# Step 2's W_in split placed behind step 1's activations, and the last two units' value products placed behind step 0's seventh product

## The chip, the cores and the metric

The kernel runs on one core of a Trainium2 chip. The metric is the device time of one execution in microseconds (us), the median of several runs. Its engines are called PE (TensorE, matmuls), ACT (ScalarE), DVE (VectorE), POOL (GpSimd) and SP (SyncE, which here only issues transfers).

## The reference

Three parts follow each other, all in fp32.

1. Banded attention: 2 batches x 8 heads, 768 positions, head size 64. A query sees the first 8 positions and the last 96 up to itself, with a distance bias; softmax; product with V.
2. `x1 = silu(x @ W_in) @ W_out` on 1536 tokens, model width 512, hidden width 2048.
3. `x2 = (h * clip(h + 3, 0, 6) / 6) @ W_out2` with `h = x1 @ W_in2`, same sizes. The output is 1536 x 512.

## The kernel before, in words

Every engine has its own hand-written list of instructions, executed in that order; semaphores order the lists against each other. An instruction that waits holds up all that stands behind it on its engine.

**Attention.** Eight pairs of heads x 6 query tiles give 48 *units* (`NU = 48`). For a unit PE computes scores (`scores`, line 901), DVE subtracts and finds the maximum, ACT exponentiates, POOL multiplies by the inverse sum, PE transposes (`turn_probs`, 911), DVE or ACT copies the transposed tile out of PSUM (`copy_t`), and PE multiplies with V (`values`, 926). `values(u)` waits for the copy of unit `u`. Every third unit ACT copies the result into `x_raw` (`x_copy`, 702; the last one, `x_copy(15)`, waits for `values` of units 45 to 47).

**The two feed-forward layers.** There are 32 *steps* (`NSTEP`): four blocks (layer, batch) of 8 steps, each step handling 256 of 2048 hidden columns for 768 tokens. In a step the product with W_in is done by a seven-product (Winograd form of Strassen's) scheme: POOL makes four sums of quarters of the weights (`w_sum`, lines 300, 302, 305, 308), and PE runs the products in the order P1, P2, P6, P5, P7, P3, P4 (`product`, line 954). Every fp32 operand is cut into a high part (ACT, a copy to fp32r) and a low part (DVE, a subtraction), and each product is 6 matmuls of 128x384: hi x hi, lo x hi, hi x lo, for two halves of the depth. So a step has 42 of them. Two PSUM banks hold the partial results (`p_bank`):

- `keep` (ACT, line 728) copies P1 out to `p1_c`, P6 to `u2_c`, P5 to `p5_c`. P6 waits for `p1_c`; P7, which adds into the bank that `u2_c` is read from, waits for `u2_c`; P3 waits for `p5_c`.
- `c_sum` (DVE, 478) adds such a copy to a bank: first after P2, then after P7, then after P3. P5 waits for the first, P4 for the second.
- `gated` (ACT, 740) takes the sigmoid of four quarters, `silu` (DVE, 488) multiplies; `g_high` (ACT, 821) and `g_low` (DVE, 607) cut the result in two; `down` (PE, 1022 and 1023) multiplies with W_out in 48 matmuls per step, one step later: after the products of step `s` PE runs `down(s-1, 0)` and `down(s-1, 1)`.
- `w_high(s, part)` (ACT, 709, 128x896) and `w_low(s, part)` (DVE, 463) cut the weights of step `s` and their sums, in two parts. `w_high(s, .)` waits for all four `w_sum`s of its step. P1 of step `s` waits for the second `w_low(s, 1)` and for the four `silu`s of the step before. The load of the weights of step `s + 2` (SP) waits for `w_low(s, 1)` too.
- `wo_high` (ACT, 748) and `wo_low` (POOL, 336, 128x1024) cut W_out. POOL's list after attention is `wo_low(0)`, which waits for the fourth `silu` of step 0, `w_sum` of step 2 (four), `w_sum` of step 3 (four), `wo_low(1)`, `w_sum` of step 4, `wo_low(2)`, and so on.

**The places that the change touches.** Steps 0 and 1 have their weights cut during attention. Step 2 is the first one whose weights are cut in the general loop, and its first part stands by itself: behind `keep(1, p1_c)` on ACT (`w_high(2, 0)`), and behind `g_low(0, 1)` on DVE (`w_low(2, 0)`). The second parts stand behind the activations of step 1. In the function `banded` of PE the end of attention is woven into step 0:

```
turn_probs(NU - 1)
values(NU - 2)
for n in range(P6, P4 + 1):
    product(0, n)
values(NU - 1)
```

Of the kernel before, what the change touches and what calls it, by code (L numbers as in the profile page):

```python
# [16 lines left out]
NU = NPAIR * NT  # L17
# [41 lines left out]
def at_least(eng, sem, value):  # L59

    if isinstance(value, int) and value <= 0:
        return
    eng.wait_ge(sem, value)


def build(nc, qT, kT, v, w_in1, w_out1, w_in2, w_out2, counts, out):
    outer = ExitStack()
    with outer:
# [72 lines left out]
        def o_bank(g): return ps[:, g % 2, 0:TB]  # L141
# [254 lines left out]
        def _(dve):  # L396
# [62 lines left out]
            def w_low(s, part):  # L459

                at = slice(7 * P * part, 7 * P * part + 7 * P)
                dve.wait_ge(wi_hi_ok, 2 * s + part + 1)
                nc.vector.tensor_tensor(wi_lo[:, s % 2, at], wi_raw[:, s % 2, QC + 7 * P * part:QC + 7 * P * part + 7 * P],  # L463
                                        wi_hi[:, s % 2, at], ALU.subtract).then_inc(wi_lo_ok, 1)
# [9 lines left out]
            def c_sum(s, i, bank, add, product):  # L474

                dve.wait_ge(p_done, 7 * s + product + 1)
                dve.wait_ge(kept, 3 * s + {0: 1, 1: 3, 2: 3}[i])
                nc.vector.tensor_tensor(c_sb[:, i, :], p_bank(bank), add[:, :], ALU.add).then_inc(c_ok, 1)  # L478
# [5 lines left out]
            def silu(s, n):  # L484

                dve.wait_ge(gate_ok, 4 * s + n + 1)
                at_least(dve, g_hi_ok, 2 * s)
                nc.vector.tensor_tensor(g_quad(n), h_quad(n), gate[:, n, :], ALU.mult).then_inc(g_ok, 1)  # L488
# [113 lines left out]
            def g_low(s, f):  # L602

                dve.wait_ge(g_hi_ok, 2 * s + f + 1)
                src, hi, lo = g_f[:, f, :, :].rearrange("p a t -> p (a t)"), g_hi[:, s % 2, f, :], g_lo[:, s % 2, f, :]
                if s < NSTEP // 2:
                    nc.vector.tensor_tensor(lo, src, hi, ALU.subtract).then_inc(g_lo_ok, 1)
                else:
                    nc.vector.scalar_tensor_tensor(lo, src, 1.0 / 6.0, hi, ALU.mult, ALU.subtract).then_inc(g_lo_ok, 1)
# [22 lines left out]
            for s in range(1, NSTEP):  # L632
                blk, f = s // STEPS, s % STEPS
                evict = blk > 0 and f == 1
                c_sum(s, 0, 1, p1_c, P2)
                if s == 1:
                    g_low(0, 1)
                    w_low(2, 0)
                if evict:
                    w_low(s + 1, 1)  # L640
                    y_copy(blk - 1, 5)
                c_sum(s, 1, 0, p5_c, P7)
                c_sum(s, 2, 1, u2_c, P3)
                for n in range(4):
                    if s < NSTEP // 2:
                        silu(s, n)
                    else:
                        hswish(s, n)
                g_low(s, 0)
                g_low(s, 1)  # L650
                if s == 1:
                    w_low(2, 1)
                if f == STEPS - 1 and s < NSTEP - 1:
                    for i in range(7):
                        x_low(blk + 1, i)
                if s + 2 < NSTEP:
                    w_low(s + 2, 0)
                    if blk > 0 and f == 0:
                        y_copy(blk - 1, 1)
                        y_copy(blk - 1, 3)  # L660
                    else:
                        w_low(s + 2, 1)
# [7 lines left out]
        def _(act):  # L670
# [33 lines left out]
            def w_high(s, part):  # L704

                at = slice(7 * P * part, 7 * P * part + 7 * P)
                act.wait_ge(ws_ok, 4 * s + 4)
                at_least(act, p_done, 7 * (s - 1))
                nc.scalar.activation(wi_hi[:, s % 2, at], wi_raw[:, s % 2, QC + 7 * P * part:QC + 7 * P * part + 7 * P],  # L709
                                     ACT.Copy).then_inc(wi_hi_ok, 1)  # L710
# [130 lines left out]
            for s in range(1, NSTEP):  # L841
                blk, f = s // STEPS, s % STEPS
                evict = blk > 0 and f == 1
                keep(s, p1_c, 0, P1)
                if s == 1:
                    w_high(2, 0)
                if evict:
                    w_high(s + 1, 1)
                    y_copy(blk - 1, 2)
                if s > 1:  # L850
                    wo_high(s)
                keep(s, u2_c, 0, P6)
                keep(s, p5_c, 1, P5)
                if evict:
                    y_copy(blk - 1, 4)
                for n in range(4):
                    gated(s, n)
                g_high(s, 0)
                g_high(s, 1)
                if s == 1:  # L860
                    w_high(2, 1)
                if f == STEPS - 1 and s < NSTEP - 1:
                    for i in range(7):
                        x_high(blk + 1, i)
                if s + 2 < NSTEP:
                    w_high(s + 2, 0)
                    if blk > 0 and f == 0:
                        y_copy(blk - 1, 0)
                    else:
                        w_high(s + 2, 1)  # L870
# [7 lines left out]
        def _(pe):  # L878
# [36 lines left out]
            def values(u):  # L915
                it, t = u // NT, u % NT
                if u % 3 == 0:
                    at_least(pe, x_ok, u // 3 - 1)
                if t == 0:
                    pe.wait_ge(v_in[it % 2], 16 * (it // 2 + 1))  # L920
                pe.wait_ge(*copied(u))
                o = o_bank(u // 3)
                for a in range(0 if t else 1, 2):
                    for h in range(2):
                        vv = v_raw[it % 2][:, h, t if a else NT + t - 1, :]
                        mm = nc.tensor.matmul(o[D * h:D * h + D, P * (t % 3):P * (t % 3) + P], vv,  # L926
                                              probsT[:, u % 2, 2 * h + a, :], start=(a == 0 or t == 0), stop=(a == 1))
                mm.then_inc(pv_done, 1)

            def product(s, n):  # L930

                a, b, bank = PRODUCTS[n]
                if n == P1:
                    pe.wait_ge(wi_lo_ok, 2 * s + 2)
                    at_least(pe, g_ok, 4 * s)
                elif n == P2:
                    at_least(pe, c_ok, 3 * s)
                elif n == P6:
                    pe.wait_ge(kept, 3 * s + 1)
                elif n == P5:  # L940
                    pe.wait_ge(c_ok, 3 * s + 1)
                elif n == P7:
                    pe.wait_ge(kept, 3 * s + 2)
                elif n == P3:
                    pe.wait_ge(kept, 3 * s + 3)
                elif n == P4:
                    pe.wait_ge(c_ok, 3 * s + 2)
                if s % STEPS == 0:
                    pe.wait_ge(x_lo_ok, 7 * (s // STEPS) + b + 1)
                fresh = n in (P1, P2, P5)  # L950
                for k in range(2):
                    at = slice(QC * a + P * k, QC * a + P * k + P)
                    for i, (w, x) in enumerate(((wi_hi, x_hi), (wi_lo, x_hi), (wi_hi, x_lo))):
                        mm = nc.tensor.matmul(p_bank(bank), w[:, s % 2, at], x[:, b, k, :],  # L954
                                              start=fresh and k == 0 and i == 0, stop=k == 1 and i == 2,
                                              skip_group_check=True)
                mm.then_inc(p_done, 1)

            def banded():
                for u in range(NU):  # L960
                    scores(u)
                    if u >= LAG:
                        turn_probs(u - LAG)
                    if u >= LAG + 1:
                        values(u - LAG - 1)
                values(NU - 6)
                turn_probs(NU - 5)
                pe.wait_ge(neg_done, 2 * NU)
                product(0, P1)
                turn_probs(NU - 4)  # L970
                values(NU - 5)
                product(0, P2)
                turn_probs(NU - 3)
                values(NU - 4)
                turn_probs(NU - 2)
                values(NU - 3)
                turn_probs(NU - 1)
                values(NU - 2)
                for n in range(P6, P4 + 1):
                    product(0, n)  # L980
                values(NU - 1)

            def general():
# [84 lines left out]
            s = NSTEP - 1  # L1068
# [53 lines left out]
```

## Time and profile before

| | |
|---|---|
| median of 3 runs | 608.09 us (607.88 to 610.44) |
| the profiled execution, its own time | 607.72 us |
| its span, first to last instruction | 606.0 us |
| mean granted PE clock | 0.997 |
| PE busy | 594.7 us (98%) |
| DVE busy | 369.2 us (61%) |
| ACT busy | 341.6 us (56%) |
| POOL busy | 284.1 us (47%) |

Times in the trace count from the start of the span. Attention reaches to about 95 us, step 0 lies between 88 and 101 us, step 1 from 102.7 us; from there on the steps follow each other, and PE is busy in nearly all of each slice.

### The profile page before, as it was taken

What the parts mean: (1) busy time and instruction counts of PE and PEld (TensorE: products, weight loads), DVE (VectorE), ACT (ScalarE), POOL (GpSimd) and SP (SyncE); (2) the same over time, 40 slices, a digit from 0 to 9 for tenths busy, and PEclk for the clock granted to TensorE, in tenths of its full rate; (3) what the DMA queues carried; (4) which work ended last, traced back from release to release, by engine and by line L of the source; (5) the groups of instructions that cost most, each with busy time, mean ns of one, the idle gap of its engine ahead of it and who ended that gap; (6) DMA issues with size and microseconds to landing.
All of it is one profiled execution on the core that took longest, in us unless ns stands there. A gap on an engine that the chain in (4) does not pass through costs nothing.

```text
span 606.0 us, 9614 instructions
## 1 busy us (share of the span) xinstructions
PE 594.7 (98%) x3429; PEld 516.4 (85%) x3429; DVE 369.2 (61%) x696; ACT 341.6 (56%) x659; POOL 284.1 (47%) x353
## 2 busy tenths in 40 slices
PE   8999999799999999999999999999999999999998
PEld 5665568799999999999999998888888988898896
DVE  6678886655755568557555865575557685554331
ACT  6889885544454466444444675545447565555441
POOL 4787995656933314439433144394333343331110
PEclk9999999899999999999999999999999999999999
DMA  8435330032222113221211123212221252221002
GB/s 351 162 110 206 110 117 5 34 138 70 71 70 70 70 35 105 70 69 37 88 59 64 38 70 101 71 36 104 70 69 36 70 175 70 69 70 35 1 1 104
DMA packets 14595, 50.05 MB, mean 83 GB/s; under 512 B 1618, under 2 KB 1874, under 8 KB 14546
## 3 DMA queue, kind: packets, MB, share of 16 engines
q1 hardware_dynamic: 14258, 48.63, 23.4%
q10 hardware_dynamic: 288, 0.79, 0.4%
q8 instruction: 28, 0.46, 0.3%
q14 instruction: 21, 0.17, 0.1%
HBM read 46.27 MB, written 3.15 MB: 82 GB/s over the span
## 4 chain that ended last, share of the span: by engine, by line
PE 88%; POOL 6%; ACT 2%; DVE 2%; issue 1%; DMA 0%; DVEq 0%; ACTq 0%
PE ps L954 38%; PE ps L1031 22%; PE ps L1022 14%; PE ps L1023 8%; POOL probs L291 3%; PE ps L926 2%; PE ps L911 2%; PE ps L901 2%; POOL rsume L283 1%; ACT probs L680 1%; POOL wo_lo L336 0%; POOL x_t L323 0%; POOL x_t L328 0%; DVE x_lo L472 0%; DVE g_f L488 0%
## 5 line engine op out<-in xcount | busy, mean ns | idle before, releaser
L336 POOL TENSOR_TENSOR wo_lo<-wo_raw,wo_hi 128x1024 fp32r<-128x1024 f32 x32 | 76.6, 2395 | 265.7 <-ACT wo_hi L748 258.3
L954 PE MATMUL ps<-x_hi,wi_hi 128*128 128x384 f32 x448 | 151.6, 338 | 4.1 <-ACT u_c L728 3.1
L954 PE MATMUL ps<-x_hi,wi_lo 128*128 128x384 f32 x448 | 150.6, 336 | 0.0
L954 PE MATMUL ps<-x_lo,wi_hi 128*128 128x384 f32 x448 | 150.4, 336 | 0.0
L478 DVE TENSOR_TENSOR c_sb<-ps,p_c 128x384 f32<-128x384 f32 x64 | 35.6, 557 | 166.4 <-PE ps L954 166.1
L728 ACT ACTIVATE p_c<-ps 128x384 f32<-128x384 f32 x64 | 31.5, 492 | 132.3 <-PE ps L954 132.1
L954 PEld LDWEIGHTS ps<-x_hi,wi_hi 128*128 128x128 f32 x448 | 84.6, 189 | 8.0 <-ACT u_c L728 4.3
L954 PEld LDWEIGHTS ps<-x_hi,wi_lo 128*128 128x128 f32 x448 | 84.5, 189 | 0.7
L954 PEld LDWEIGHTS ps<-x_lo,wi_hi 128*128 128x128 f32 x448 | 84.5, 189 | 0.0
L1031 PE MATMUL ps<-wo_hi,g_lo 128*128 128x512 f32 (+1 forms) x194 | 76.3, 393 | 0.0
L1031 PE MATMUL ps<-wo_lo,g_hi 128*128 128x512 f32 (+1 forms) x194 | 76.3, 393 | 0.0
L1031 PE MATMUL ps<-wo_hi,g_hi 128*128 128x512 f32 (+1 forms) x194 | 76.2, 393 | 0.0
L463 DVE TENSOR_TENSOR wi_lo<-wi_raw,wi_hi 128x896 fp32r<-128x896 f32 x64 | 72.4, 1166 | 3.1 <-ACT wi_hi L709 3.1
L821 ACT ACTIVATE g_hi<-g_f 128x768 fp32r<-128x768 f32 x64 | 50.6, 838 | 37.1 <-DVE g_f L488 21.3
L709 ACT ACTIVATE wi_hi<-wi_raw 128x896 fp32r<-128x896 f32 x64 | 57.4, 938 | 4.9 <-POOL wi_raw L308 4.9
L1022 PE MATMUL ps<-g_hi,wo_hi 128*128 128x512 f32 x128 | 50.0, 391 | 0.0
L1022 PE MATMUL ps<-g_lo,wo_hi 128*128 128x512 f32 x128 | 50.0, 391 | 0.0
L1022 PE MATMUL ps<-g_hi,wo_lo 128*128 128x512 f32 x128 | 50.0, 390 | 0.0
L680 ACT ACTIVATE probs<-negs,negmax 128x256 f32<-128x256 f32 (+1 forms) x96 | 45.9, 481 | 5.5 <-DVE negmax L499 5.2
L291 POOL TENSOR_SCALAR probs<-probs,rinv 128x256 f32<-128x256 f32 (+1 forms) x96 | 45.3, 485 | 4.1
L499 DVE CUSTOM_DVE_ANT_0 negs<-ps,m_bias 128x256 f32<-128x256 f32 (+1 forms) x96 | 37.3, 391 | 14.7 <-PE ps L901 12.1
L1031 PEld LDWEIGHTS ps<-wo_hi,g_lo 128*128 128x128 f32 x194 | 36.4, 188 | 8.6
(94 smaller groups left out, 1091.0 us busy)
## 6 DMA issues: line engine op xcount, KB each, us to landing
wi_raw<-in_w_in SPq DMA_DIRECT2D x32, 512.0 KB, 3.3
wo_raw<-in_w_out SPq DMA_DIRECT2D x32, 512.0 KB, 3.4
v_raw<-in_v SPq DMA_DIRECT2D x8, 704.0 KB, 4.2
k_raw<-in_kT SPq DMA_DIRECT2D x8, 464.0 KB, 5.0
out_y<-y_out SPq DMA_DIRECT2D x11, 256.0 KB, 4.4
q_raw<-in_qT SPq DMA_DIRECT2D x6, 384.0 KB, 5.5
q_raw<-in_qT ACTq DMA_DIRECT2D x2, 384.0 KB, 4.0
out_y<-y_out SPq DMA_DIRECT2D x2, 128.0 KB, 1.9
```

The costliest lines, as they stand in the source:

```text
L291: nc.gpsimd.tensor_scalar(probs[:, u % DEEP, h, a:256], probs[:, u % DEEP, h, a:256], rinv[:, u % DEEP, h:h + 1], 1.0, ALU.mult, ALU.mult) ...
L336: nc.gpsimd.tensor_tensor(wo_lo[:, s % 2, :], wo_raw[:, s % 2, :], wo_hi[:, s % 2, :], ALU.subtract).then_inc(wo_lo_ok, 1)
L463: nc.vector.tensor_tensor(wi_lo[:, s % 2, at], wi_raw[:, s % 2, QC + 7 * P * part:QC + 7 * P * part + 7 * P], wi_hi[:, s % 2, at], ALU.sub ...
L478: nc.vector.tensor_tensor(c_sb[:, i, :], p_bank(bank), add[:, :], ALU.add).then_inc(c_ok, 1)
L499: nc.vector.tensor_tensor_reduce(negs[:, u % 2, h, 0 if t else P:256], sc, bi, -0.125, 3.0e38, ALU.add, ALU.min, negmax[:, u % DEEP, h:h + ...
L680: nc.scalar.activation(probs[:, u % DEEP, h, a:256], negs[:, u % 2, h, a:256], ACT.Exp, bias=negmax[:, u % DEEP, h:h + 1], scale=-1.0, acc ...
L709: nc.scalar.activation(wi_hi[:, s % 2, at], wi_raw[:, s % 2, QC + 7 * P * part:QC + 7 * P * part + 7 * P], ACT.Copy).then_inc(wi_hi_ok, 1)
L821: nc.scalar.activation(g_hi[:, s % 2, f, :], g_f[:, f, :, :].rearrange("p a t -> p (a t)"), ACT.Copy, scale=1.0 if s < NSTEP // 2 else 1.0 ...
L954: mm = nc.tensor.matmul(p_bank(bank), w[:, s % 2, at], x[:, b, k, :], start=fresh and k == 0 and i == 0, stop=k == 1 and i == 2, skip_grou ...
L1022: nc.tensor.matmul(y_bank(i), wo[:, s % 2, w], g[:, s % 2, c, 0:512], start=first, stop=last)
L1023: mm = nc.tensor.matmul(y_bank(4 + i // 2)[:, 256 * (i % 2):256 * (i % 2) + 256], wo[:, s % 2, w], g[:, s % 2, c, 512:S], start=first and ...
L1031: mm = nc.tensor.matmul(y_bank(t)[:, cols], g[:, s % 2, c, P * t:P * t + P], wo[:, s % 2, DM * c + cols.start:DM * c + cols.stop], start=s ...
```

## The change

On ACT `w_high(2, 0)`, and on DVE `w_low(2, 0)`, move from the middle of step 1 to behind the `g_high`s and `g_low`s of step 1, directly ahead of `w_high(2, 1)` and `w_low(2, 1)`. On PE `values(46)` moves from ahead of P6 of step 0 to behind P4 of step 0, ahead of `values(47)`. Nothing is added or removed.

```
@@ DVE
                 c_sum(s, 0, 1, p1_c, P2)
                 if s == 1:
                     g_low(0, 1)
-                    w_low(2, 0)
...
                 g_low(s, 0)
                 g_low(s, 1)
                 if s == 1:
+                    w_low(2, 0)
                     w_low(2, 1)
@@ ACT
                 keep(s, p1_c, 0, P1)
-                if s == 1:
-                    w_high(2, 0)
...
                 g_high(s, 0)
                 g_high(s, 1)
                 if s == 1:
+                    w_high(2, 0)
                     w_high(2, 1)
@@ PE, banded
                 turn_probs(NU - 1)
-                values(NU - 2)
                 for n in range(P6, P4 + 1):
                     product(0, n)
+
+                values(NU - 2)
                 values(NU - 1)
```

ACT in steps 0 and 1 (`g_high` of step 0 first; p_c is `p1_c` or `p5_c`, u_c is `u2_c`):

```order
 L821 ACTIVATE g_hi<-g_f 128x768 x2
 L728 ACTIVATE p_c<-ps 128x384
-L709 ACTIVATE wi_hi<-wi_raw 128x896
-L728 ACTIVATE u_c<-ps 128x384
-L728 ACTIVATE p_c<-ps 128x384
-L740 ACTIVATE gate<-c_sb 128x384 x3
-L740 ACTIVATE gate<-ps 128x384
-L821 ACTIVATE g_hi<-g_f 128x768 x2
-L709 ACTIVATE wi_hi<-wi_raw 128x896 x3
+L728 ACTIVATE u_c<-ps 128x384
+L728 ACTIVATE p_c<-ps 128x384
+L740 ACTIVATE gate<-c_sb 128x384 x3
+L740 ACTIVATE gate<-ps 128x384
+L821 ACTIVATE g_hi<-g_f 128x768 x2
+L709 ACTIVATE wi_hi<-wi_raw 128x896 x4
```

The copies `u2_c` and `p5_c` of step 1 now come directly behind `p1_c`, and four weight cuts (two for step 2, two for step 3) follow step 1's `g_high`s instead of three.

DVE in step 1, from its first `c_sum` on:

```order
 L478 TENSOR_TENSOR c_sb<-ps,p_c 128x384
 L607 TENSOR_TENSOR g_lo<-g_f,g_hi 128x768
-L463 TENSOR_TENSOR wi_lo<-wi_raw,wi_hi 128x896
-L478 TENSOR_TENSOR c_sb<-ps,p_c 128x384
-L478 TENSOR_TENSOR c_sb<-ps,u_c 128x384
-L488 TENSOR_TENSOR g_f<-c_sb,gate 128x384 x3
-L488 TENSOR_TENSOR g_f<-ps,gate 128x384
-L607 TENSOR_TENSOR g_lo<-g_f,g_hi 128x768 x2
-L463 TENSOR_TENSOR wi_lo<-wi_raw,wi_hi 128x896 x3
+L478 TENSOR_TENSOR c_sb<-ps,p_c 128x384
+L478 TENSOR_TENSOR c_sb<-ps,u_c 128x384
+L488 TENSOR_TENSOR g_f<-c_sb,gate 128x384 x3
+L488 TENSOR_TENSOR g_f<-ps,gate 128x384
+L607 TENSOR_TENSOR g_lo<-g_f,g_hi 128x768 x2
+L463 TENSOR_TENSOR wi_lo<-wi_raw,wi_hi 128x896 x4
```

The subtraction for step 2's first part leaves the place ahead of step 1's second `c_sum` and stands first of four behind the `g_low`s.

## Rows read from the trace of the kernel before

**Rows 1.** Waits of PE, whole span: line, releaser, us in total, times, longest us
```profile
PE ps L954 <- ACT u_c L728: 3.1, 1, 3.1
PE ps L911 <- POOL probs L291: 2.3, 7, 0.7
...
PE ps L954 <- DVE g_f L488: 0.7, 1, 0.7
...
PE ps L954 <- DVE c_sb L478: 0.3, 1, 0.3
```

**Rows 2.** Timeline of PE: start us, us, line, operation, [idle before, releaser]
```profile
103.80 0.33 PE L954 MATMUL ps<-x_hi,wi_hi 128*128 128x384 f32 x1
...
106.35 0.44 PE L954 MATMUL ps<-x_hi,wi_hi 128*128 128x384 f32 x1 [0.31 <-DVE c_sb L478]
...
110.72 0.69 PE L954 MATMUL ps<-x_hi,wi_hi 128*128 128x384 f32 x1 [3.05 <-ACT u_c L728]
...
115.32 0.39 PE L1022 MATMUL ps<-g_hi,wo_hi 128*128 128x512 f32 x1
...
123.66 0.34 PE L954 MATMUL ps<-x_hi,wi_hi 128*128 128x384 f32 x1
```

**Rows 3.** Timeline of ACT, steps 0 and 1
```profile
102.00 0.49 ACT L702 ACTIVATE x_raw<-ps 128x384 f32<-128x384 f32 x1
103.99 0.49 ACT L728 ACTIVATE p_c<-ps 128x384 f32<-128x384 f32 x1
109.34 0.95 ACT L709 ACTIVATE wi_hi<-wi_raw 128x896 fp32r<-128x896 f32 x1 [4.85 <-POOL wi_raw L308]
110.20 0.47 ACT L728 ACTIVATE u_c<-ps 128x384 f32<-128x384 f32 x1
```

**Rows 4.** Timeline of POOL, steps 0 to 1
```profile
102.61 2.40 POOL L336 TENSOR_TENSOR wo_lo<-wo_raw,wo_hi 128x1024 fp32r<-128x1024 f32 x1 [7.35 <-DVE g_f L488]
104.97 1.44 POOL L300 TENSOR_TENSOR wi_raw<-wi_raw 128x256 f32<-128x256 f32 x1
108.58 0.72 POOL L308 TENSOR_TENSOR wi_raw<-wi_raw 128x256 f32<-128x256 f32 x1
```

**Rows 5.** Busy time of each engine by stretch (100 to 120 us)
```profile
105.00:110.00 5.00, 2.36 (x12) 1.72 (x11) 2.23 (x3) 0.66 (x1) 4.92 (x7) 1.00 0.30 105
110.00:115.00 5.00, 4.28 (x17) 4.28 (x18) 2.37 (x4) 1.99 (x5) 4.92 (x4) 0.66 0.00 0
```

**Rows 6.** Timeline of PE, end of step 0
```profile
101.02 0.34 PE L954 MATMUL ps<-x_lo,wi_hi 128*128 128x384 f32 x1
101.29 0.66 PE L926 MATMUL ps<-probsT,v_raw 128*64 128x128 f32 x8
102.68 0.41 PE L954 MATMUL ps<-x_hi,wi_hi 128*128 128x384 f32 x1 [0.73 <-DVE g_f L488]
```

**Rows 7.** Timeline of DVE, end of step 0 and step 1
```profile
101.98 0.55 DVE L488 TENSOR_TENSOR g_f<-ps,gate 128x384 f32<-128x384 f32 x1
103.32 2.50 DVE L607 TENSOR_TENSOR g_lo<-g_f,g_hi 128x768 fp32r<-128x768 f32 x1 [0.79 <-ACT g_hi L821]
105.75 0.55 DVE L478 TENSOR_TENSOR c_sb<-ps,p_c 128x384 f32<-128x384 f32 x1
```

**Rows 8.** Timeline of DVE, from the last matmuls of step 1
```profile
114.96 1.76 DVE L488 TENSOR_TENSOR g_f<-c_sb,gate 128x384 f32<-128x384 f32 x3
119.37 3.09 DVE L463 TENSOR_TENSOR wi_lo<-wi_raw,wi_hi 128x896 fp32r<-128x896 f32 x3
130.57 2.33 DVE L488 TENSOR_TENSOR g_f<-c_sb,gate 128x384 f32<-128x384 f32 x3
```

**Rows 9.** By source line: duration ns min/median/max, first and last start us
```profile
L607 DVE TENSOR_TENSOR g_lo<-g_f,g_hi x32: 946/959/2504, 103.3 to 338.1; 128x768 fp32r<-128x768 f32 x32
L488 DVE TENSOR_TENSOR g_f<-c_sb,gate x48: 544/736/1375, 99.8 to 335.7; 128x384 f32<-128x384 f32 x48
L463 DVE TENSOR_TENSOR wi_lo<-wi_raw,wi_hi x64: 1075/1085/1904, 38.7 to 559.6; 128x896 fp32r<-128x896 f32 x64
```

More of the change, by code:

```diff
@@ L637, in _ @@
                     g_low(0, 1)
-                    w_low(2, 0)
                 if evict:
@@ L651, in _ @@
                 if s == 1:
+                    w_low(2, 0)
                     w_low(2, 1)
@@ L844, in _ @@
                 keep(s, p1_c, 0, P1)
-                if s == 1:
-                    w_high(2, 0)
                 if evict:
@@ L860, in _ @@
                 if s == 1:
+                    w_high(2, 0)
                     w_high(2, 1)
@@ L977, in banded @@
                 turn_probs(NU - 1)
-                values(NU - 2)
                 for n in range(P6, P4 + 1):
                     product(0, n)
+                values(NU - 2)
                 values(NU - 1)
```

## Prediction

> **What bounds the kernel now.** I read the totals first: PE is busy 98% of the span, the next engine 61%. So the end is set by PE's list, and a change can only matter through PE's idle time, its clock, or new waits. The list of PE's waits comes next [rows 1]. It is short. The largest single wait of the whole run is one of 3.1 us: a matmul of the W_in products that waits for ACT's copy `u2_c`. One of 0.7 us waits for a `silu`. The 2.3 us at line 911 are seven small waits inside attention, which the change doesn't touch.
>
> The timeline of PE puts the long wait into step 1 [rows 2]. P2 of step 1 starts at 103.80, P5 at 106.35, and the next product, P7, only at 110.72. ACT shows why [rows 3]: `u2_c` needed only P6, whose six matmuls ended at about 106.0, but its copy ran at 110.20, because `w_high(2, 0)` stood ahead of it in ACT's list, ran at 109.34, and had itself been waiting 4.85 us for POOL. POOL had begun only at 102.61, with `wo_low(0)`, and finished the fourth sum of step 2 at 108.58 + 0.72 = 109.30 [rows 4]. So the chain is POOL, `w_high(2, 0)`, `u2_c`, P7, and nobody needs `w_high(2, 0)` before P1 of step 2, at 123.66 [rows 2].
>
> The view by stretches adds a second cost [rows 5]: in 105 to 110 us PE works 2.36 of 5 us at granted clock 1.00; in 110 to 115 us the clock is 0.66 on average, full (2.4 GHz) for part and half (1.2 GHz) for part. The stretch that follows the idle time is run partly at the low level.
>
> **Edit A, `w_high(2, 0)` and `w_low(2, 0)` moved.** Three terms.
>
> 1. The idle time. P5 to P7 takes 110.72 - 106.35 = 4.37 us. Six matmuls at the usual distance take 1.04 us (P2 started 1.04 us before P6), 1.15 us with the slower first one behind a wait. Gain: 4.37 - 1.15 = 3.2 us. Is anything else late at P7? `u2_c` now follows P6 directly, as ACT has nothing between: about 106.1 to 106.6, ahead of P7's new turn. P3 wants `p5_c`, a copy of 0.49 us behind P5, with a whole product for it. P4 wants the second `c_sum`, one product after P7; DVE is free by then, since `w_low(2, 0)` has left that place as well.
> 2. The clock. From P7 to the first `down` matmul there are 18 matmuls: 115.32 - 110.72 = 4.60 us [rows 2]. At 1.04 us for six they take 3.12 us. Gain: 1.5 us, since with no long idle time there is nothing that the clock would fall after.
> 3. What the moved work costs in its new place. Two instructions: 0.95 us on ACT [rows 3], 1.08 us on DVE [rows 9]. PE's next use is P1 of step 2, which waits for `w_low(2, 1)`. Between P4 of step 1 and P1 of step 2 PE has `down` of step 0: 123.66 - 115.32 = 8.34 us [rows 2]. Before, DVE came to `w_low(2, 1)` at 119.37 and ended it about 1.03 us later (3.09 us for three) [rows 8], that is 120.4, or 5.1 us behind the start of `down`. With one more subtraction it is 6.1 us: 2.2 us before PE asks. That is the bound with no loss.
>
> But term 3 has a second bound. DVE's subtractions and products that read two SBUF tiles stretch where POOL is at work: `g_low` takes 0.96 us in the median and took 2.50 us at 103.32, ending at 105.82, 0.8 us behind the end of `wo_low(0)` at 105.0 [rows 4, 7]; the `silu`s go up to 1.38 us from 0.54, and `w_low` to 1.90 from 1.08 [rows 9]. Additions that read PSUM keep 0.55 us. With step 1 now ending five microseconds earlier, its `silu`s and `g_low`s fall on POOL's sums for step 3 and on `wo_low(1)`, which before ran mostly while DVE was idle. I lay POOL's list out from its new start (edit B): `wo_low(0)` at 102.0, sums of step 2 to 108.7, sums of step 3 to about 112.1 (two of them held up by DVE), `wo_low(1)` (2.40 us) to about 114.9. DVE: `silu`s from 109.7 in about 2.8 us (2.33 us for three in step 2, under the same kind of load [rows 8]), the fourth to 113.0, ACT's `g_high`s to 114.2. The first `g_low` then waits for `wo_low(1)` to end, as it did for `wo_low(0)`: 115.7; the second 116.5; two `w_low`s to 118.5 to 118.8. PE would be ready for P1 at 110.0 + 8.34 = 118.4. I take a wait of **0.3 us**, since the layout leaves it between 0 and 0.6. If every one of the seven SBUF-only operations (three `silu`, two `g_low`, two `w_low`) were stretched as far as the longest rows [rows 9], it would be 3 x 0.83 + 2 x 1.54 + 2 x 0.82 = 7.2 us, a wait of 5 us, and the low clock once more behind it. That is the far bound, and it is not near: POOL has only one 2.4 us operation there.
>
> The Trainium skill ("SBUF — State Buffer", section "Who interferes with whom") says that a DVE instruction with two SBUF inputs and a GpSimd instruction that reads SBUF take one shared port in turn, each for its whole length. The trace agrees: `g_low` at 103.32 ended 0.8 us after `wo_low(0)` did. It is this rule that speaks against the change; without it the wait at P1 would be nil and the sum 0.3 us better.
>
> **What else hangs on the moved operations.** The load of step 4's weights follows `w_low(2, 1)`; before, that ended 3.2 us ahead of step 2's P1, now at about the same time as P1. So POOL gets to the sums of step 4 and to `wo_low(2)` some 3 us later within step 2, where the `silu`s of step 2 meet them. The first user is P1 of step 4, two steps later, and `down(2)`, over a step later; I cost it at nothing. The cover is POOL's idle time, about half the span (47% busy).
>
> **Edit B, `values(46)` behind P4.** It takes 0.59 us of PE's time wherever it stands: the last P4 matmul starts at 101.02, `values(47)` at 101.29 and ends at 101.95, and P1 of step 1 at 102.68 after 0.73 us of waiting for the fourth `silu` of step 0, which ran 101.98 to 102.53 [rows 6, 7]. With `values(46)` behind the products, all five products and the `silu`s that follow them come 0.59 us earlier; the `silu` ends at 101.94, `values(47)` at 101.95 as before. P1 starts at 102.1. The wait was swapped for work: 0.6 us. Does it last? Not all of the way on ACT: `x_copy(15)` still waits for `values(47)`, so it stays at 102.00, and `p1_c` of step 1 behind it at 103.99 [rows 3]. P6 waits for that to 104.6 (P2 ends at 104.2). The next gate is P5, which waits for the `c_sum` at 105.75 on DVE [rows 7]. It stood behind the long `g_low`, and this one behind `wo_low(0)` on POOL, which is released by the very `silu` that comes 0.59 us earlier. So P5 starts at 105.8 for 106.35: **0.6 us**, with 0.1 us to spare at P6. Bounds: 0 (P6 or ACT takes it) and 0.7.
>
> **Sum.** 3.2 + 1.5 + 0.6 - 0.3 = 5.0 us. The profiled execution took 607.72 us with a span of 606.0; it becomes 602.7 with a span of 601.0. The median of the runs shown is 0.37 us above the profiled one, so I forecast 608.09 - 5.0 = **603.1 us**. After P1 of step 2 everything moves along: the list of waits holds none of PE that the next steps would bring back [rows 1].
>
> **Rivals.**
>
> 1. *The port takes more.* POOL's `wo_low(1)` catches a `silu` as well as a `g_low`, or the `w_low`s too, and P1 of step 2 waits 1 to 2.5 us. For: the stretched rows [rows 9]; against: one such operation in the window. Gain 5.3 - 1.8 = 3.5, 604.6 us (603.8 to 605.3).
> 2. *Edit B is swallowed.* `x_copy(15)` and the copies behind it hold up P6 so that P5 is not earlier. Gain 4.4, 603.7 us. The range holds it.
> 3. *The low clock was not in the timed runs.* The clock fell in the profiled execution after 3.2 us of idling. If it did not in the median run, that run can only gain the idle time: 3.2 + 0.6 - 0.3 = 3.5 us, 604.6. For: nothing in the rows; against: its time agrees with the median within 0.1%. The Trainium skill ("TensorE: Matmul & The Clock Gate", section "What's actually happening") says that the point of transition depends on where in the monitor's window the matmuls fall and varies from run to run; no single trace can show it.
> 4. *Slower.* P1 of step 2 waits so long that PE loses the clock there. Place: `w_low(2, 1)`, behind ACT's four cuts and the stretched DVE operations. Price: the wait plus 1.5 us. It decides from 3.8 us of waiting on, as 3.8 + 1.5 = 5.3: `w_low(2, 1)` ending later than 122.2. The far bound of 5 us gives 608.09 - 5.3 + 6.5 = 609.3. For it: only the far bound; against it: in my layout it ends at 118.5 to 118.8.
> 5. *The change doesn't do what it says.* Something else releases P7 late, so that the idle time stays. Against: `u2_c` ran directly behind `w_high(2, 0)`, with P6 4 us done. Then only edit B is left: 607.5 us.
>
> **How the numbers follow.** Forecast (with rival 2 in its range) 0.75, rival 1 0.12, rival 3 0.06, rival 4 0.03, rival 5 0.04. A measurement of this kernel can tell about 0.5%, 3.0 us, from no change. Faster by more than that is below 605.05: the forecast, rival 3 and most of rival 1, 0.91. Within 0.5%: the rest of rival 1, rival 5, some of rival 4, 0.07. Slower by more than 0.5% (over 611.1): 0.02. The range runs from 602.0 (no wait at P1, 0.7 from edit B, and 0.7 us of spread between runs) to 605.3, where rival 1 ends.
>
> **What would show it.** In the profile of the changed kernel: no wait of PE for `u2_c` at step 1, and granted clock 1.00 from 105 to 115 us; P5 of step 1 at 105.8, the first `down` matmul at 110.0, for 106.35 and 115.32; a new short wait of PE for `wi_lo` (DVE, line 463) at about 118.4, with `g_low` of step 1 stretched beside `wo_low(1)`; and no new one later. Wrong: a wait over 1 us there (rival 1), a clock below 1 around 120 us (rival 4), or P7 still behind P5 by more than 1.2 us (rival 5).

## The result and the profile after

The changed kernel took 604.42 us (median of 11 runs, 602.71 to 606.27), the kernel before in the same set 608.14 us (11 runs, 606.59 to 610.57); the ratio is 0.9927, with a 95% interval of 0.9908 to 0.9946. That is 3.7 us between the medians, 4.4 us by the ratio. The profiled execution took 604.96 us, with a span of 603.2 us and a mean granted clock of 0.994. The forecast was 603.1 us, with a range of 602.0 to 605.3.

The waits of PE in the changed kernel, whole span (line, releaser, us in total, times, longest):

```profile
PE ps L910 <- POOL probs L291: 2.8, 6, 1.4
PE ps L884 <- POOL ident L276: 1.4, 1, 1.4
PE ps L900 <- DVE negmax L499: 1.2, 3, 0.7
PE ps L900 <- DMA k_raw<-in_kT: 0.4, 1, 0.4
PE ps L953 <- DVE g_f L488: 0.3, 1, 0.3
```

The wait of 3.1 us for `u2_c` [rows 1] is gone, and the 0.7 us for the `silu` is 0.3. The 1.2 us at line 900 (scores) is new; it lies in early attention, where the change does nothing, and is taken up below.

PE's timeline (line 953 is 954 of before), in the places of [rows 2, 6]:

```profile
102.91 1.10 PE L925 MATMUL ps<-probsT,v_raw 128*64 128x128 f32 x16
104.29 0.41 PE L953 MATMUL ps<-x_hi,wi_hi 128*128 128x384 f32 x1 [0.29 <-DVE g_f L488]
...
107.98 0.44 PE L953 MATMUL ps<-x_hi,wi_hi 128*128 128x384 f32 x1
...
109.13 0.33 PE L953 MATMUL ps<-x_hi,wi_hi 128*128 128x384 f32 x1
...
112.25 0.39 PE L1022 MATMUL ps<-g_hi,wo_hi 128*128 128x512 f32 x1
...
120.84 0.44 PE L953 MATMUL ps<-x_hi,wi_hi 128*128 128x384 f32 x1
```

These are both `values`, then P1, P5 and P7 of step 1, `down` of step 0, and P1 of step 2. P7 follows P5 after 1.15 us (4.37 before), `down` follows P7 after 3.12 us (4.60 before). P1 of step 2 stands 8.59 us behind the start of `down`, for 8.34 before: the new wait, 0.25 us. The granted clock is 1.00 in every stretch from 100 to 125 us.

ACT, DVE and POOL in step 1 [rows 3, 4, 7, 8]:

```profile
105.99 0.47 ACT L728 ACTIVATE p_c<-ps 128x384 f32<-128x384 f32 x1
107.88 0.49 ACT L728 ACTIVATE u_c<-ps 128x384 f32<-128x384 f32 x1 [1.42 <-PE ps L953]
...
116.34 3.46 ACT L709 ACTIVATE wi_hi<-wi_raw 128x896 fp32r<-128x896 f32 x4
```

```profile
105.38 2.07 DVE L607 TENSOR_TENSOR g_lo<-g_f,g_hi 128x768 fp32r<-128x768 f32 x1 [1.24 <-ACT g_hi L821]
107.38 0.55 DVE L478 TENSOR_TENSOR c_sb<-ps,p_c 128x384 f32<-128x384 f32 x1
...
111.88 2.94 DVE L488 TENSOR_TENSOR g_f<-c_sb,gate 128x384 f32<-128x384 f32 x3
114.74 0.55 DVE L488 TENSOR_TENSOR g_f<-ps,gate 128x384 f32<-128x384 f32 x1
115.73 3.06 DVE L607 TENSOR_TENSOR g_lo<-g_f,g_hi 128x768 fp32r<-128x768 f32 x2 [0.44 <-ACT g_hi L821]
118.71 4.08 DVE L463 TENSOR_TENSOR wi_lo<-wi_raw,wi_hi 128x896 fp32r<-128x896 f32 x4
```

```profile
104.23 2.41 POOL L336 TENSOR_TENSOR wo_lo<-wo_raw,wo_hi 128x1024 fp32r<-128x1024 f32 x1 [6.57 <-DVE g_f L488]
...
114.37 2.73 POOL L336 TENSOR_TENSOR wo_lo<-wo_raw,wo_hi 128x1024 fp32r<-128x1024 f32 x1
```

`u2_c` waits for PE now, not for a place in ACT's list. On DVE the three `silu`s take 2.94 us and the two `g_low`s 3.06 us beside POOL's sums and `wo_low(1)`, which itself is stretched from 2.40 to 2.73 us. The second `w_low` ends at about 118.71 + 2.06 = 120.77, and P1 follows at 120.84.

So the places that the change touches look as forecast, yet the span is 603.2 us and not 601.0. Where the rest went shows in the first 20 us. The stretches 10 to 15 and 15 to 20 us, of before and of after (PE, PEld, DVE, ACT and POOL busy, granted clock, DMA):

```profile
10.00:15.00 5.00, 4.11 (x26) 2.03 (x24) 3.64 (x21) 5.00 (x22) 3.24 (x10) 1.00 1.03 410
15.00:20.00 5.00, 5.00 (x50) 3.13 (x46) 3.35 (x17) 4.30 (x15) 3.72 (x11) 1.00 0.47 180
```

```profile
10.00:15.00 5.00, 3.56 (x16) 1.85 (x16) 2.31 (x15) 4.76 (x21) 3.35 (x10) 0.68 1.02 411
15.00:20.00 5.00, 5.00 (x29) 2.93 (x28) 2.69 (x11) 2.45 (x8) 3.17 (x8) 0.63 0.44 168
```

In the profiled execution of the changed kernel the clock was at its lower level for part of early attention, and PE got through 29 instructions in the second stretch where it did 50 before. P1 of step 0 starts at 91.09 us, against 88.69 before. That is 2.4 us which no instruction of the change explains: up to there both kernels run the same list.

The two executions differ from the first scores on. Before:

```profile
5.48 6.17 PE L901 MATMUL ps<-k_raw,q_raw 64*128 64x256 f32 x24 [0.31 <-DMA k_raw<-in_kT]
```

After:

```profile
5.57 1.14 PE L900 MATMUL ps<-k_raw,q_raw 64*128 64x256 f32 x8 [0.41 <-DMA k_raw<-in_kT]
...
12.14 0.69 PE L910 MATMUL ps<-ident,probs 128*128 128x128 f32 x2 [1.40 <-POOL probs L291]
12.77 1.22 PE L900 MATMUL ps<-k_raw,q_raw 64*128 64x256 f32 x4
```

In the changed kernel's execution the first scores ran faster, PE then had to wait for DVE's `negmax` (the 1.2 us at line 900) and for POOL, and the clock fell at about 12 us. In the execution of before the scores ran slowly without a gap, and no fall came.

This gives a cleaner measure: the time from P1 of step 0 to the end of the span. It was 606.0 - 88.69 = 517.3 us before and 603.2 - 91.09 = 512.1 us after, 5.2 us less. (Spans are given to 0.1 us, so this measure is good to about that.)

### The profile page after: what moved, and what is told of

The parts are those of the page before. It is cut to its first block, busy times and chain, and to the rows that moved or that the text cites. A ratio compares the mean times of both kernels' runs of the same rounds, so it can differ in the third digit from the quotient of the medians.

```text
span 603.2 us, 9614 instructions
## 1 busy us (share of the span) xinstructions
PE 593.7 (98%) x3429; PEld 515.2 (85%) x3429; DVE 373.6 (62%) x696; ACT 341.5 (57%) x659; POOL 284.3 (47%) x353
## 4 chain that ended last, share of the span: by engine, by line
PE 89%; DVE 4%; POOL 3%; ACT 2%; issue 1%; DMA 0%; DVEq 0%; ACTq 0%
PE ps L953 38%; PE ps L1031 22%; PE ps L1022 14%; PE ps L1023 7%; PE ps L910 3%; PE ps L900 3%; PE ps L925 3%; POOL probs L291 2%; ACT probs L680 1%; POOL rsume L283 1%; DVE g_lo L607 1%; DVE wi_lo L463 1%; DVE g_f L488 0%; DVE x_lo L472 0%; POOL x_t L328 0%
```

## The experiments

The theory was the prediction's sum: 3.2 us of idle time and 1.5 us of lower clock in step 1 (edit A), 0.6 us at the seam of attention (edit B), 0.3 us given back at P1 of step 2; and, from the profile after, that early attention varies from execution to execution for reasons of its own. The rivals were that the two edits need each other, that the slow matmuls of step 1 have another cause than the wait, that DVE's half of edit A matters, and that P1 of step 2 had slack left.

The profiled execution of each kernel gives the same measures (us; the start of the first matmul of the product named, from the PE timeline):

| kernel | P1 of step 0 | P1 of step 1 | P5 | P7 | P1 of step 2 | span | span less P1 of step 0 |
|---|---|---|---|---|---|---|---|
| before | 88.69 | 102.68 | 106.35 | 110.72 | 123.66 | 606.0 | 517.3 |
| changed | 91.09 | 104.29 | 107.98 | 109.13 | 120.84 | 603.2 | 512.1 |
| changed, again | 88.90 | 102.10 | 105.78 | 106.96 | 118.62 | 601.0 | 512.1 |
| edit A alone | 89.15 | 103.12 | 106.80 | 107.97 | 119.63 | 602.0 | 512.9 |
| edit B alone | 88.98 | 102.19 | 105.87 | 110.25 | 123.39 | 605.7 | 516.7 |
| `w_low` half of A | 91.82 | 105.77 | 109.44 | 113.81 | 126.93 | 609.2 | 517.4 |
| before, wait filled | 88.69 | 102.64 | 106.31 | 110.68 | 122.27 | 604.5 | 515.8 |
| before, early fill | 92.93 | 106.88 | 110.56 | 114.92 | 128.90 | 611.2 | 518.3 |
| changed, early fill | 89.07 | 102.26 | 105.94 | 107.12 | 118.78 | 601.2 | 512.1 |
| changed, `w_low` delayed | 88.75 | 101.94 | 105.61 | 106.76 | 120.48 | 604.8 | 516.1 |
| changed, POOL reordered | 91.17 | 104.37 | 107.57 | 108.61 | 121.07 | 603.5 | 512.3 |
| changed, POOL spaced | 90.11 | 103.30 | 106.50 | 107.53 | 118.99 | 601.9 | 511.8 |

P1 of step 0 moves between 88.7 and 92.9 us, and not with the edits: the changed kernel has 91.09 in one execution and 88.90 in another. The last column is steady: 512.1 twice for the changed kernel. Steadier still is the time from P1 of step 2 to the end, 482.3 us before (606.0 - 123.66) and 482.4 in both executions of the changed kernel, so that all of the 5.2 us lies between P1 of step 0 and P1 of step 2.

**Edit A alone.** The four hunks on DVE and ACT of the change, with the values left in place.

> Edit A alone: the two weight cuts of step 2 moved, the values left where they were. My theory (three terms: idle time 3.2 us, low clock 1.5 us, a short wait at P1 of step 2 of 0.2 us): P7 of step 1 follows P5 within 1.2 us, the first down matmul of step 0 comes 4.7 us earlier relative to P5, and the time is 4.4 us below the kernel before when early attention runs at the same clock in both. A rival, that the two edits only work together (the cuts moved without the earlier silu leave POOL's sums late for something else), would show another wait of PE in step 1 and less than 3 us of gain.

Measured: 603.71 us (6 runs, 603.31 to 606.09), before 609.13 (22 runs), ratio 0.9914 (0.9893 to 0.9936). By the last column 517.3 - 512.9 = 4.4 us, as expected. P7 follows P5 after 1.17 us. The edit works by itself; the rival falls. The medians are 5.4 us apart, more than for the whole change, because four of the six runs had the quick start (mean clock 1.000); the last column is free of that.

**Edit B alone.** The hunk on PE of the change.

> Edit B alone: values of unit 46 behind P4, the cuts left in place. My theory: P1 of step 1 starts 0.6 us earlier, and POOL's list too, so that w_high(2, 0), u2_c and P7 all come 0.6 us earlier (P7 is released by POOL's chain, which starts at the fourth silu): 0.6 us less in all, the low clock of step 1 stays. The rival, that x_copy(15) and p1_c hold it back: less than 0.2 us. In the timed comparison neither can be told from nothing; the trace tells.

Measured: 607.34 us (11 runs, 606.94 to 610.47), ratio 0.9975 (0.996 to 0.999). By the last column 0.6 us less. `x_copy(15)` did not hold it back. P1 of step 1 still waits 0.3 us for the `silu`, where the prediction had no wait left. P7 is still late:

```profile
102.19 0.41 PE L954 MATMUL ps<-x_hi,wi_hi 128*128 128x384 f32 x1 [0.29 <-DVE g_f L488]
105.87 0.44 PE L954 MATMUL ps<-x_hi,wi_hi 128*128 128x384 f32 x1 [0.15 <-DVE c_sb L478]
110.25 0.45 PE L954 MATMUL ps<-x_hi,wi_hi 128*128 128x384 f32 x1 [3.07 <-ACT u_c L728]
```

From P1 of step 0 to P5 it saves 17.66 - 16.89 = 0.77 us, a little more than the 0.6 forecast: besides the 0.59 us of `values(46)`, P6 starts 0.41 us behind the start of the last transposes, where `values(46)` started 0.58 us behind it. At P7 there is 22.03 - 21.27 = 0.76 us; behind P7 the lower clock comes at another place, and 0.6 is left at the end.

**The wait filled with other work.** On PE, between P5 and P7 of step 1 of the kernel before:

```
                     for n in range(7):
                         product(s, n)
+                        if s == 1 and n == P5:
+                            for _ in range(18):
+                                nc.tensor.transpose(ps[:, 2, 0:P], ident[:, :], ident[:, :])
```

> The kernel before, order untouched, with 18 unused 128x128 transposes on PE between P5 and P7 of step 1, into a bank that nothing reads at that time. They fill 2.7 us of the 3.1 us in which PE waits for u2_c, and change nothing of the wait itself. My theory (the wait costs 1.5 us more than its own length, because the clock falls after it): P7 still starts 4.4 us behind P5, but the 18 matmuls from P7 to the first down matmul take 3.1 to 3.2 us instead of 4.6, granted clock 1.00 in 105 to 120 us, and the fastest runs are 1.3 to 1.5 us below the fastest of the kernel before. The rival, that the slow matmuls have another cause (transfers, the pile-up of copies on ACT and DVE): 4.6 us as before and no gain.

Measured: 607.44 us (12 runs, 606.21 to 609.16), before 608.86 (23 runs, 606.43 to 612.11), ratio 0.9982 (0.9965 to 0.9998). The wait stands, 1.1 us of it unfilled, and the clock stays up:

```profile
110.68 0.45 PE L954 MATMUL ps<-x_hi,wi_hi 128*128 128x384 f32 x1 [1.10 <-ACT u_c L728]
```

```profile
105.00:110.00 5.00, 4.28 (x30) 3.69 (x28) 2.18 (x3) 0.70 (x1) 4.92 (x6) 1.00 0.30 105
110.00:115.00 5.00, 4.32 (x25) 4.19 (x26) 3.76 (x4) 2.89 (x7) 4.92 (x4) 1.00 0.01 3
```

The 18 transposes filled 2.0 us, less than the 2.7 expected. P7 starts 4.37 us behind P5, to the hundredth as before, so nothing of the wait itself was removed; from P7 to `down` it is 113.94 - 110.68 = 3.26 us for 4.60, and the last column falls by 1.5 us. This is the clock [rows 5], the second term of edit A, measured by itself: 1.3 us up to `down`, 1.5 us at the end. The fastest run, 606.21 us, is only 0.2 us below the fastest of before in this set (606.43) and 1.3 us below the next (607.55). The run also gives the span that the kernel before has when it keeps the clock in step 1: 604.5 to 604.7 us. Five of the 12 filled runs have that, and one of the 23 of before, 604.6 us at a mean clock of 0.999; in all sets together two of 67 runs of before took less than 607 us. Other runs of before may have kept the clock in step 1 and lost it in early attention: the filled kernel then has spans of 605.6 to 606.0 us, which can't be told from before with the loss in step 1 (605.8 to 606.3).

**DVE's half of edit A.** Only `w_low(2, 0)` moved on DVE, `w_high(2, 0)` left on ACT.

> Half of edit A: only DVE's w_low(2, 0) moved behind the g_lows of step 1, ACT's w_high(2, 0) left in the middle of step 1. My theory (ACT's list is what holds P7: u2_c stands behind w_high(2, 0)): P7 still 4.4 us behind P5, PE's 3.1 us wait for u2_c stays. From P7 on, DVE's second c_sum of step 1 comes 0 to 0.3 us sooner; no other difference. The rival, that DVE's subtraction was part of the hold-up: P7 or P4 a microsecond earlier.

Measured: one execution only, 610.95 us, span 609.2 with a late start of step 0 at 91.82; the last column is 517.4 for 517.3. PE still waits 3.05 us for `u2_c`:

```profile
113.81 0.44 PE L954 MATMUL ps<-x_hi,wi_hi 128*128 128x384 f32 x1 [3.05 <-ACT u_c L728]
```

P7 is 4.37 us behind P5. So DVE's half does nothing by itself, and what holds P7 is in ACT's list. ACT's half alone was not run: `w_low(2, 0)` waits for `w_high(2, 0)`, so DVE would then stand at its old place until the cut was made.

**P1 of step 2 delayed.** The changed kernel with, on DVE:

```
                 if s == 1:
                     w_low(2, 0)
+                    for j in range(2):
+                        nc.vector.tensor_tensor(y_out[:, 2 * j:2 * j + 2, 0:448],
+                                                wi_raw[:, 0, QC:QC + 7 * P].rearrange("p (a k) -> p a k", a=2),
+                                                wi_raw[:, 0, QC:QC + 7 * P].rearrange("p (a k) -> p a k", a=2), ALU.subtract)
                     w_low(2, 1)
```

> The changed kernel with two unused subtractions of 128x896 on DVE (1.02 us each, results into the output buffer, overwritten at the end) between w_low(2, 0) and w_low(2, 1). My theory (P1 of step 2 is now released by w_low(2, 1), with no slack left): P1 of step 2 starts 2.0 us later than in the changed kernel, PE waits 2.2 us for DVE line 463, and the time rises by 2.0 us, or by up to 3.5 if the clock falls behind the wait. The rival, that P1 had slack of about 2 us and the 0.2 us gap there was something else: no wait over 0.5 us and the time unchanged.

Measured: 605.84 us (10 runs, 604.89 to 607.81), ratio to before 0.995 (0.9928 to 0.9972). The profile shows the wait with its name, and the clock that went with it:

```profile
120.48 0.69 PE L957 MATMUL ps<-x_hi,wi_hi 128*128 128x384 f32 x1 [2.10 <-DVE wi_lo L463]
```

```profile
120.00:122.00 2.00, 1.52 (x5) 1.52 (x6) 2.00 (x3) 0.00 (x0) 0.00 (x0) 0.62 0.28 109
122.00:124.00 2.00, 2.00 (x8) 2.00 (x7) 0.43 (x1) 1.20 (x2) 0.43 (x1) 0.53 0.87 336
```

From P1 of step 0 to P1 of step 2 it is 31.73 us, for 29.72 to 29.75 in the changed kernel: the added 2.0 us in full. So `w_low(2, 1)` is what releases P1, without slack. Five of the ten runs kept the clock (mean 1.000) and have spans of 603.1 to 603.4 us, 2.1 to 2.4 over the 601.0 of the changed kernel at that clock. The profiled one lost it behind the wait, and paid 516.1 - 512.1 = 4.0 us in all, more than the 3.5 that I had set as the upper end: the lower clock took 2.0 us here. So a wait of 2 us costs the clock in some executions and not in others.

**Early attention filled.** For the kernel before, and the same for the changed one:

```
                 for u in range(NU):
                     scores(u)
+                    if 1 <= u < 5:
+                        busy(2)
+                    if u == 5:
+                        busy(6)
```

> The kernel before with added PE work in early attention: two unused 128x128 transposes behind the scores of units 1 to 4, six behind those of unit 5, all into a bank that nothing reads yet. They fill idle time of PE between 7 and 12 us. My theory on the spread between runs (602.7 to 606.3 for the changed kernel, by the mean granted clock 1.000 to 0.994): in some executions the clock falls to its lower level in early attention, where PE idles, which has nothing to do with the change. With the idle time filled it should stay high: runs no longer at 610 us, median 606.5 to 608. The rival, that the spread comes from elsewhere: the same spread and median as the kernel before, or up to 1 us more for the added work.

> The changed kernel with the same added PE work in early attention. My theory: nearly all runs at the level of the fastest of the changed kernel, 602.7 us, with clock 1.000; the difference to the kernel before with the same filling is then the whole of the forecast, 4.5 to 5.2 us (less if that one loses no clock in step 1 in its median run: then 3.7). The rival: 604.4 us with the old spread.

Measured: 609.38 us for before with the filling (12 runs, 607.5 to 613.17), ratio 1.0004 (0.9983 to 1.0026); 604.3 us for the changed kernel with it (6 runs, 602.93 to 606.92), ratio 0.9925 (0.9899 to 0.995). The spread did not shrink, it grew, and in the profiled execution of before P1 of step 0 came later than in any other (92.93). My idea of the cause fell, at least as I had put it, that idle time there makes the clock fall. The profile of before with the filling shows slow scores, as in the first microseconds of before without it:

```profile
7.71 0.69 PE L885 MATMUL ps<-ident 128*128 128x128 f32 x2
8.33 1.23 PE L901 MATMUL ps<-k_raw,q_raw 64*128 64x256 f32 x4
```

Four score matmuls take 1.23 us here until about 18 us, with PE busy without a gap from 8 to 18 us, and 0.70 us from 18.8 us on. In the changed kernel's first profile four take 1.22 us at 12.77 us, where the clock column says 0.50. So by its matmul durations PE ran at the low level here with no idle time from the first scores on, though the clock column says 1.00. The six runs of the changed kernel with the filling show the same: all have a mean clock of 1.000, and spans from 601.2 to 605.2 us. The last column of the changed kernel is unmoved by it, 512.1 us once more. That of before is 518.3, 1.0 us more than without the filling, since the lower clock lasted longer in step 1: 5.66 us from P7 to `down`, for 4.60.

**POOL reordered.** The changed kernel; on ACT `x_copy(15)` goes behind the two `g_high`s of step 0, and on POOL:

```
             pool.wait_ge(g_ok, 4)
-            wo_low(0)
             for s in range(NSTEP):
                 ...
-                if s:
+                if s == 0:
+                    wo_low(0)
+                    wo_low(1)
+                if s > 1:
                     wo_low(s)
```

> The changed kernel with two reorderings that aim at the waits that are left. On POOL the four sums of step 2 go ahead of wo_low(0), and wo_low(1) directly behind wo_low(0), ahead of the sums of step 3. On ACT x_copy(15) goes behind the two g_highs of step 0. My theory (the shared SBUF port makes g_low wait for the long wo_low): g_low(0, 0) of 2.07 us shrinks below 1.7 us, P5 of step 1 starts within 3.2 us of P1 (3.69 in the changed kernel), and the gap ahead of P1 of step 2 goes away: 0.5 to 0.7 us less in all, which the timed runs can hardly tell. The rival, that the wait only moves: four short sums hold up DVE as long as one long subtraction, or down of step 0 now waits for wo_low(0) or x_copy(15): no gain, a new wait of PE at about 110 us.

Measured: 605.04 us (6 runs, 604.3 to 605.38), ratio 0.9939 (0.9916 to 0.9962); last column 512.3, no gain. The first half came true, the second turned over. `g_low(0, 0)` shrank to 1.19 us and P5 stands 3.20 us behind P1. But the two long subtractions now stand back to back where the `silu`s of step 1 are due:

```profile
104.66 1.19 DVE L609 TENSOR_TENSOR g_lo<-g_f,g_hi 128x768 fp32r<-128x768 f32 x1 [0.44 <-ACT g_hi L756]
...
111.36 4.54 DVE L490 TENSOR_TENSOR g_f<-c_sb,gate 128x384 f32<-128x384 f32 x3
```

```profile
108.71 4.75 POOL L336 TENSOR_TENSOR wo_lo<-wo_raw,wo_hi 128x1024 fp32r<-128x1024 f32 x2
```

```profile
121.07 0.44 PE L957 MATMUL ps<-x_hi,wi_hi 128*128 128x384 f32 x1 [0.85 <-DVE wi_lo L465]
```

Three `silu`s take 4.54 us for 2.94, and PE waits 0.85 us at P1 of step 2. The rival (the wait only moves) was right, though not at the place it named.

**POOL spaced.** As the last one, but with `wo_low(1)` in its old place behind the sums of step 3, and a wait ahead of it:

```
+                if s == 1:
+                    pool.wait_ge(wi_lo_ok, 6)
+                wo_low(s)
```

> The changed kernel with x_copy(15) behind the g_highs of step 0 (ACT), the four sums of step 2 ahead of wo_low(0) (POOL), and wo_low(1) held back until w_low(2, 1) is done, in place of directly behind the sums of step 3. My theory (DVE's chain of silu, g_low and w_low in step 1 is stretched by POOL's long subtractions only while they overlap it): P5 of step 1 3.1 us behind P1 (3.69 in the changed kernel), the two g_lows of step 1 at 1.9 us together (3.06), no wait of PE at P1 of step 2, and P1 of step 1 to P1 of step 2 in 15.9 to 16.0 us for 16.55; in all 0.5 to 0.6 us less than the changed kernel, which is at the edge of what five rounds can tell. The rival, that wo_low(1) or the sums of step 4, now later, hold up step 2: a new wait of PE between 121 and 135 us, no gain.

**The changed kernel again,** on the same chip.

> The changed kernel once more, on the same chip as the run above, for the comparison. Runs at clock 1.000 at a span of 601.0 to 601.2, 0.997 at 602.3 to 602.7, 0.994 at 603.2 to 603.5; the kernel before at 0.997 at 605.8 to 606.2: a difference of 4.9 to 5.0 us between executions whose early attention went alike.

Measured: 603.71 us for the spaced one (5 runs, 603.64 to 604.7), ratio 0.9925 (0.9909 to 0.994), and 603.39 us for the changed kernel (6 runs, 602.73 to 605.45), ratio 0.9923 (0.9903 to 0.9942), with before at 608.88 (11 runs). In the trace the spaced one does nearly what it should: the two `g_low`s of step 1 take 1.83 us, P1 of step 2 has no wait and comes 15.69 us behind P1 of step 1 (16.52 in the changed kernel). Half of that is then lost at P5 of step 2, since the last `w_low` of step 3 meets the delayed `wo_low(1)`, which is the rival's new wait behind 121 us:

```profile
114.08 1.83 DVE L607 TENSOR_TENSOR g_lo<-g_f,g_hi 128x768 fp32r<-128x768 f32 x2 [0.45 <-ACT g_hi L754]
115.82 6.29 DVE L463 TENSOR_TENSOR wi_lo<-wi_raw,wi_hi 128x896 fp32r<-128x896 f32 x4
```

```profile
122.64 0.44 PE L955 MATMUL ps<-x_hi,wi_hi 128*128 128x384 f32 x1 [0.36 <-DVE c_sb L478]
```

Four `w_low`s in 6.29 us for 4.08. The last column is 511.8 for 512.1, 0.3 us better for the 0.5 to 0.6 expected; the medians can't tell the two apart. It is no version to prefer on what was measured.

## Why the prediction was right, point by point

- **Idle time, 3.2 us.** P5 to P7 went from 4.37 to 1.15 us: 3.2. P7 had been held by ACT's list, as read from [rows 3]; the `w_low` half alone did nothing.
- **Lower clock, 1.5 us.** P7 to `down` went from 4.60 to 3.12 us, and filling the wait gave 1.3 us of this up to `down` (1.5 at the end) with the wait left in place. The size is that of one execution: the other three profiles with the wait unfilled have 4.70, 4.82 and 5.66 us there, so this term can be 1.3 to 2.4 us against the filled kernel's 3.26.
- **Given back at P1 of step 2, 0.3 us.** Measured 0.25. The lay-out held well: `silu`s 2.94 us (2.8 laid out), `g_low`s stretched by `wo_low(1)`, `w_low(2, 1)` the releaser. The delayed kernel shows that no slack is left there.
- **Edit B, 0.6 us.** Measured 0.8 at P5 and 0.6 at the end when alone; together with edit A it adds 512.85 - 512.1, about 0.7 us. The prediction had counted only the 0.59 us of `values(46)`; that it came out near the end's 0.6 when alone is partly chance, since behind P7 the clock took 0.2 back.
- **Nothing lost later, POOL's delay costed at nothing.** No wait of PE behind 121 us is in the list of the changed kernel, and from P1 of step 2 to the end it takes 482.4 us for 482.3.
- **The sum, 5.0 us.** Measured from P1 of step 0 on, 5.2 us, and the second profiled execution has the span that was forecast, 601.0 us, with P5 of step 1 at 105.78, `down` at 110.08 and P1 of step 2 at 118.62, for 105.8, 110.0 and 118.7.

What the prediction mis-sized is the last step, from the profiled execution to the median: "0.7 us of spread between runs", and the start of the program taken as fixed. The three runs of before that it had already reached from 607.88 to 610.44 us. The time until P1 of step 0 differs by 2.4 us between the profiled executions of before and after, and by up to 3.1 us over the profiles of kernels without added work in attention (88.69 to 91.82). The 11 runs of the changed kernel had mean clocks of 1.000 twice, 0.997 four times and 0.994 five times, with spans around 601.05, 602.5 and 603.6 us; by its mean clock of 0.997 its median run had the lower clock for part of early attention, while the profiled execution of before on which the sum was built had no such fall.

Two profiled executions without that fall can be compared directly: 606.0 us before (P1 of step 0 at 88.69) and 601.0 us for the changed kernel, again (88.90), which is 5.0 us. Over all sets, before averages 609.1 us (67 runs) and the changed kernel 604.3 us (17 runs), 4.8 us apart. The first set's medians show 3.7 because they fell on different sides: only two of the 11 runs of the changed kernel were quick ones (602.7 to 602.8 us), while six of the 11 of before took 608.2 us or less, for 15 of 56 in the other sets, whose medians of before are 608.9 to 609.1. That 604.42 us still lay inside the range owes something to luck: the room above the forecast was held for rival 1, not for the start.

Rival 1 (the port takes more), rival 4 (slower) and rival 5 (P7 still late) did not occur, nor did rival 2 (edit B swallowed); the kernel with POOL reordered shows that rival 1's mechanism is real, with 0.85 us of wait at the very place. Rival 3 named a time near the measured one, 604.6, for another reason: that before keeps its clock in step 1. The profiled execution lost it, and only two of 67 runs are so fast that they must have kept it; for many of the others the times alone don't tell. That the time came out near it is the start's doing.

## What to carry to other kernels

A short wait of the engine that bounds a kernel can cost much more than its length through the clock: 1.5 us on top of 3.1 us here, and 2.0 us on top of 2.0 in the delayed kernel. To price removing it, read the matmuls behind it as well as the gap, and to test that share alone, fill the gap with unused work. When one instruction waits in front of a copy that a busy engine needs, look at what it waits for, and when its own result is first needed: here a weight cut needed 14 us later stood ahead of a copy needed at once. And compare executions from a point behind the start-up, not only by their totals, when an effect is below 1%.

## What the runs showed of the hardware that was not expected

- The clock of the first 20 us varies by execution. In four of the ten profiles without added work in attention it fell at about 12 to 13 us, behind PE's wait of 1.2 to 1.4 us for POOL; in the other six that wait was 0.7 to 1.3 us. Both executions whose first eight scores took 1.14 us had the fall, and the five whose first 20 or more scores ran without a gap had none. Filling PE's gaps with 128x128 transposes did not keep the start quick: in one execution PE was busy for all of 8 to 18 us and still took 1.23 us for four score matmuls that take 0.70 at the high level. The column of granted clock reads 1.00 in that stretch; the matmul durations tell the level there (1.22 us for four at a column of 0.50), not the column. What decides it stays open; no run here isolates it.
- A wait of 2.1 us lost the clock in the profiled execution of the delayed kernel and did not in five other runs, whose mean clock is 1.000. All four profiled executions with the wait of 3.0 to 3.1 us unfilled lost it (before, edit B alone, the `w_low` half, before with early fill).
- POOL's subtraction is stretched by DVE's as well as the other way round: `wo_low(1)` took 2.73 us beside the `silu`s and 3.18 us beside the `w_low`s in the spaced kernel, for 2.40 alone. There the rows of the two engines show turns: a `w_low` that began at 117.83 us ended at 118.91; `wo_low(1)` ended 2.26 us behind that; the next `w_low` 0.95 us behind `wo_low(1)`.

```profile
117.99 3.18 POOL L336 TENSOR_TENSOR wo_lo<-wo_raw,wo_hi 128x1024 fp32r<-128x1024 f32 x1 [4.23 <-DVE wi_lo L463]
```

```profile
118.83 3.29 DVE L463 TENSOR_TENSOR wi_lo<-wi_raw,wi_hi 128x896 fp32r<-128x896 f32 x1
```

The Trainium skill ("SBUF — State Buffer", section "Who interferes with whom") has it that whichever starts first holds the port and the other blocks; these rows agree.
